# Attention and two feed-forward layers: one copy per product group out of PSUM, its halves joined by a DMA and GpSimd, and other waits in the first pair

## What is computed

```python
# q, k, v: (2, 8, 768, 64) f32; proj: (64, 6)
q_bits = (einsum('bhsd,dk->bhsk', q, proj) > 0); k_bits likewise
mask   = q_bucket[:, :, :, None] == k_bucket[:, :, None, :]   # same 6 bits
scores = where(mask, q @ k.T / 8, -1e9)
attn   = exp(scores - max); attn = attn / (sum(attn) + 1e-9)
x      = (attn @ v)  -> (1536, 512)            # heads side by side
# feed-forward 1: h = x @ w_in; g = P(h) / (Q(|h|) + 1e-6); x = g @ w_out    (512 -> 2048 -> 512)
# feed-forward 2: h = x @ w_in; g = h - tanh(h);            x = g @ w_out
```

## Time and profile before

| | |
|---|---|
| median of 3 runs | 796.71 us (795.78 to 798.22) |
| profiled execution | 797.45 us, its span 795.6 us, granted clock 0.998 of full |
| busy | PE 773.9 us (97%), DVE 554.8 (70%), ACT 476.3 (60%), POOL 127.3 (16%) |
| DMA | 56.54 MB, mean 71 GB/s; nearly all of it issued by SyncE |
| chain that ended last | PE 73%, DVE 16%, DMA 3%, issue 3% |

### The profile page before, as it was taken

One profiled execution on the slowest core, in us unless ns is written; L12 is line 12 of the kernel. 1 busy time (PEld: TensorE's weight loads), 2 busy tenths in 40 slices (PEclk: granted clock), 3 DMA queues, 4 the chain that ended last, 5 costly groups with the idle time before them and its releaser, 6 DMA issues.

```text
span 795.6 us, 11859 instructions
## 1 busy us (share of the span) xinstructions
PE 773.9 (97%) x3840; PEld 647.5 (81%) x3840; DVE 554.8 (70%) x895; ACT 476.3 (60%) x921; POOL 127.3 (16%) x112
## 2 busy tenths in 40 slices
PE   5989999999999999999999999999999999999998
PEld 3879899899988777787888888888888888888886
DVE  4869999999997999999888988966442322223222
ACT  3869889889888687877666766755432222222221
POOL 5334524533539200000000000000000000000000
PEclk9999999999999999999999999999999999999999
DMA  5766767677474430000000132320000100001001
GB/s 114 156 159 151 169 152 180 154 168 181 114 182 113 129 124 0 1 2 1 0 1 15 26 102 84 106 81 13 0 1 1 53 1 1 0 1 54 0 1 54
DMA packets 64603, 56.54 MB, mean 71 GB/s; under 512 B 31664, under 2 KB 50352, under 8 KB 64560
## 3 DMA queue, kind: packets, MB, share of 16 engines
q1 hardware_dynamic: 62848, 55.52, 27.5%
q10 hardware_dynamic: 1712, 0.46, 0.3%
HBM read 29.57 MB, written 3.19 MB: 41 GB/s over the span
## 4 chain that ended last, share of the span: by engine, by line
PE 73%; DVE 16%; DMA 3%; issue 3%; POOL 1%; SPq 1%; ACT 1%; DVEq 0%; ACTq 0%; POOLq 0%
PE acc L718 28%; PE h_ps L689 27%; PE slot L232 5%; PE turn_ps L353 5%; PE pv_ps L313 3%; PE pv_ps L315 3%; DVE sqr L824 2%; DVE row_min L501 2%; DVE pol L845 2%; DVE pt_lo L548 2%; DVE pol L837 1%; DMA kA<-k_hot 1%; DVE pol L856 1%; DVE pol L831 1%; DVE wout_lo L885 1%
## 5 line engine op out<-in xcount | busy, mean ns | idle before, releaser
L689 PE MATMUL h_ps<-x_hi,win_lo 128*128 128x512 f32 x384 | 151.6, 395 | 0.0
L689 PE MATMUL h_ps<-x_lo,win_hi 128*128 128x512 f32 x384 | 151.4, 394 | 0.0
L689 PE MATMUL h_ps<-x_hi,win_hi 128*128 128x512 f32 x384 | 151.2, 394 | 0.0
L739 ACT ACTIVATE g_hi<-pol 128x512 fp32r<-128x512 f32 x96 | 60.9, 634 | 129.5 <-PE acc L718 105.3
L869 DVE TENSOR_TENSOR g_lo<-pol,g_hi 128x512 fp32r<-128x512 f32 x96 | 65.9, 686 | 101.4 <-ACT g_hi L739 101.2
L548 DVE TENSOR_TENSOR pt_lo<-turn_ps,pt_hi 128x384 fp32r<-128x384 f32 x192 | 98.0, 551 | 12.1 <-ACT pt_hi L452 10.7
L452 ACT ACTIVATE pt_hi<-turn_ps 128x384 fp32r<-128x384 f32 x192 | 84.2, 490 | 22.9 <-PE turn_ps L353 21.8
L501 DVE TENSOR_REDUCE row_min<-slot 128x1 f32<-128x768 f32 x96 | 90.6, 944 | 6.6 <-PE slot L232 6.6
L428 ACT ACTIVATE E<-slot,row_min 128x768 f32<-128x768 f32 x96 | 87.4, 910 | 2.7 <-DVE row_min L501 2.7
L689 PEld LDWEIGHTS h_ps<-x_lo,win_hi 128*128 128x128 f32 x384 | 72.2, 188 | 16.9
L689 PEld LDWEIGHTS h_ps<-x_hi,win_hi 128*128 128x128 f32 x384 | 72.2, 188 | 16.8
(11 more groups left out here) (105 smaller groups left out, 1367.3 us busy)
## 6 DMA issues: line engine op xcount, KB each, us to landing
win_raw<-in_moe_w_in SPq DMA_DIRECT2D x32, 256.0 KB, 3.1
wout_raw<-in_moe_w_out SPq DMA_DIRECT2D x32, 256.0 KB, 2.8
q_nat<-in_q SPq DMA_DIRECT2D x16, 192.0 KB, 3.4
v_nat<-in_v SPq DMA_DIRECT2D x8, 384.0 KB, 4.6
scale<-softmax_scale SPq DMA_DIRECT2D x16, 192.0 KB, 3.1
qA<-q_hi SPq DMA_DIRECT2D x15, 192.0 KB, 2.5
qB<-q_hi SPq DMA_DIRECT2D x15, 192.0 KB, 3.0
qB<-q_lo SPq DMA_DIRECT2D x15, 192.0 KB, 3.2
```

The lines of the kernel that those rows point to most:

```text
L689: mm = eng.matmul(h_ps[t % 4][:, :], w[:, ws], columns(x, kt, c), start=kt + n == 0, stop=kt == KT - 1 and n == 2)
L739: eng.activation(g_hi[:, t % TEMPS, :], pol[:, t % TEMPS, :], ACT.Copy).then_inc(mlp_sems["g_hi"], 1)
```

## The change

Three parts. **Groups:** every group leaves `pv_ps` in one copy of 128x384, group 1 by VectorE and the others by ScalarE, into a new tile `x_raw[e]`. A DMA moves the half that stands on the wrong partitions into `x_pair` (`shift`), and GpSimd adds the other half to it (`pool_add`), for head 0 at n = 11, for head 1 at n = 3 of the next pair at the head of `pool_x`. For head 1 the high part of v now stands in the second 64 columns. **Queue:** `spread_scale` is split into `scale_out` and `scale_in`, and these and the shifts get new places in `sync_att`. **First pair:** ScalarE instead of VectorE makes the copy `opA[0][1]` of k, the loads of `ca` and `cb` have a semaphore of their own (`coefs`), which only their users wait for, and `cb_abs` moves behind the first exponentials.

```diff
         def act_first(eng):
...
+            eng.wait_ge(loads["t_k"], 2)
+            eng.activation(opA[0][1][0:D, :], turned[1][0:D, :], ACT.Copy
+                           ).then_inc(loads["t_hi_k"], 1)
-            eng.wait_ge(loads["consts"], 16 * N_CONST)
+            eng.wait_ge(loads["consts"], 32)
...
-            eng.tensor_copy(opA[0][1][0:D, :], turned[1][0:D, :]).then_inc(loads["t_hi_k"], 1)
-            eng.tensor_copy(opB[0][1][0:D, :], turned[1][0:D, :]).then_inc(loads["t_hi_k"], 1)
+            eng.tensor_copy(opB[0][1][0:D, :], turned[1][0:D, :]).then_inc(loads["t_hi_kb"], 1)
...
-        def act_pv_low(eng, p, c):
+        def group_free(eng, p, c):
             eng.wait_ge(sems["pv"], BIAS + GROUPS * p + c + 1)
-            eng.wait_ge(sems["x_sum"], BIAS + GROUPS * p + c)
-            eng.activation(pv_low[:, :], pv_ps[D:2 * D, 0:HALF], ACT.Copy
-                           ).then_inc(sems["pv_low"], 1)
+            eng.wait_ge(sems["x_add"], BIAS + 2 * p - 1 + c // 2)
+
+        def act_out(eng, p, c):
+            if c != DVE_GROUP:
+                group_free(eng, p, c)
+                eng.activation(group_at(c), pv_ps[:, 0:HALF], ACT.Copy).then_inc(sems["out_act"], 1)
...
-        def dve_x_sum(eng, p, c):
...
-            eng.tensor_tensor(x_pair[e * D:(e + 1) * D, hf * HALF:(hf + 1) * HALF],
-                              pv_ps[0:D, 0:HALF], pv_low[:, :], ALU.add
-                              ).then_inc(sems["x_sum"], 1)
+        def dve_out(eng, p, c):
+            if c == DVE_GROUP:
+                group_free(eng, p, c)
+                eng.tensor_copy(group_at(c), pv_ps[:, 0:HALF]).then_inc(sems["out_dve"], 1)
...
+        def pool_add(eng, p, e):
+            mine = slice(e * D, (e + 1) * D)
+            for c in (2 * e, 2 * e + 1):
+                done, count = group_out(p, c)
+                eng.wait_ge(done, count)
+            eng.wait_ge(loads[f"shift{e}"], 16 * (p + 1))
+            eng.sem_inc(loads["pool_here"], 1)
+            eng.tensor_tensor(x_pair[mine, :], x_pair[mine, :], x_raw[e][mine, :], ALU.add
+                              ).then_inc(sems["x_add"], 1)
...
-        def pool_x(eng, p):
+        def pool_x(eng, p, done, count):
+            eng.wait_ge(done, count)
+            pool_add(eng, p, 1)
...
+                if n == 11 and not last:
+                    pool_add(eng, p, 0)
...
+                def shift(p, e):
+                    for c in (2 * e, 2 * e + 1):
+                        done, count = group_out(p, c)
+                        eng.wait_ge(done, count)
+                        here()
+                    eng.wait_ge(sems["xn"], BIAS + p)
+                    here()
+                    eng.dma_start(x_pair[e * D:(e + 1) * D, :], x_raw[e][D - e * D:2 * D - e * D, :]
+                                  ).then_inc(loads[f"shift{e}"], 16)
...
                     copy_split(p + 1, 0)
-                    spread_scale(p, 0)
+                    if not is_zero(p):
+                        shift(p - 1, 1)
+                    scale_out(p, 0)
                     load_v(p + 1)
                     copy_hot(p + 1, 0)
+                    scale_in(p, 0)
                     copy_split(p + 1, 1)
                     copy_hot(p + 1, 1)
-                    spread_scale(p, 1)
+                    shift(p, 0)
+                    scale_out(p, 1)
+                    scale_in(p, 1)
...
-                eng.dma_start(ca[:, :], coef_a).then_inc(loads["consts"], 16)
-                eng.dma_start(cb[:, :], coef_b).then_inc(loads["consts"], 16)
+                eng.dma_start(ca[:, :], coef_a).then_inc(loads["coefs"], 16)
+                eng.dma_start(cb[:, :], coef_b).then_inc(loads["coefs"], 16)
...
                 for j in range(EARLY_OUT):
                     load_weight(0, "out", j)
-                spread_scale(PAIRS - 1, 0)
+                shift(PAIRS - 2, 1)
+                scale_out(PAIRS - 1, 0)
+                scale_in(PAIRS - 1, 0)
```

More of the change, by code:

```diff
@@ L67, in build @@
         "pe": ["pt", "pv", "scores0", "scores1", "aux"],
-        "act": ["pt_hi", "exp0", "exp1", "aux_act", "pv_low"],
-        "dve": ["rowmin", "sum", "recip", "aux_dve", "pt_lo", "x_sum"],
-        "pool": ["hi", "lo", "vhi0", "vhi1", "vlo0", "vlo1", "xn", "xhi", "xlo"],
+        "act": ["pt_hi", "exp0", "exp1", "aux_act", "out_act"],
+        "dve": ["rowmin", "sum", "recip", "aux_dve", "pt_lo", "out_dve"],
+        "pool": ["hi", "lo", "vhi0", "vhi1", "vlo0", "vlo1", "x_add", "xn", "xhi", "xlo"],
     }
@@ L75, in build @@
     loads = {name: top.enter_context(nc.semaphore("s_" + name))
-             for name in ["ident", "consts", "ready", "coef", "proj", "q", "k", "v", "out", "ops0", "ops1",
-                          "scale_out0", "scale_out1", "scale_in0", "scale_in1", "pool_here", "sync_here"]
+             for name in ["ident", "consts", "coefs", "ready", "coef", "proj", "q", "k", "v", "out", "ops0", "ops1",
+                          "scale_out0", "scale_out1", "scale_in0", "scale_in1", "shift0", "shift1", "pool_here", "sync_here"]
              + ["t_turn", "t_q", "t_k", "t_dots", "t_bits", "t_hot", "t_hot_q", "t_hot_k",
-                "t_hi_q", "t_hi_k", "t_lo"]
+                "t_hi_q", "t_hi_k", "t_hi_kb", "t_lo"]
              + [f"w_in{j}" for j in range(J)] + [f"w_out{j}" for j in range(J)]}
@@ L143, in build @@
         row_inv = sb(att, "row_inv", [P, 2, T], F32)
-        pv_low = sb(att, "pv_low", [D, HALF], F32)
+        x_raw = [sb(att, f"x_raw{e}", [P, S], F32) for e in range(2)]
         x_pair = sb(att, "x_pair", [P, S], F32)
@@ L213, in exp_done, with group_out @@
             return sems[f"exp{m % 2}"], BIAS + p * T + m // 2 + 1
+        DVE_GROUP = 1
+        def group_out(p, c):
+            if c == DVE_GROUP:
+                return sems["out_dve"], BIAS + p + 1
+            return sems["out_act"], BIAS + (GROUPS - 1) * p + (c if c < DVE_GROUP else c - 1) + 1
         def is_zero(p):
@@ L294, in pe_first @@
             eng.wait_ge(loads["t_hi_q"], 2)
-            eng.wait_ge(loads["t_hi_k"], 2)
+            eng.wait_ge(loads["t_hi_k"], 1)
+            eng.wait_ge(loads["t_hi_kb"], 1)
             eng.wait_ge(loads["t_lo"], 2)
@@ L309, in pe_pv @@
                 eng.wait_ge(sems[f"vlo{e}"], BIAS + p + 1)
-                eng.wait_ge(sems["x_sum"], BIAS + GROUPS * p + c)
+                done, count = group_out(p, c - 1) if c else group_out(p - 1, GROUPS - 1)
+                eng.wait_ge(done, count)
             for kt in range(i * T // G, (i + 1) * T // G):
@@ L404, in act_first @@
                                    ).then_inc(loads["t_hot_k"], 1)
-            eng.activation(cb_abs[:, :], cb[:, :], ACT.Abs).then_inc(loads["coef"], 1)
             for m in range(AHEAD - 1):
                 act_exp(eng, 0, m)
+            eng.wait_ge(loads["coefs"], 32)
+            eng.activation(cb_abs[:, :], cb[:, :], ACT.Abs).then_inc(loads["coef"], 1)
         def staged_free(eng, b):
@@ L555, in dve_att @@
                     dve_step(eng, 0)
-                if last and n == TILES - 2:
-                    dve_x_sum(eng, p, GROUPS - 2)
                 if first and n == 2:
@@ L704, in pe_g2 @@
                 eng.wait_ge(sems["pt_lo"], BIAS + 2 * TILES * PAIRS)
-                eng.wait_ge(sems["x_sum"], BIAS + GROUPS * PAIRS)
+                done, count = group_out(PAIRS - 1, GROUPS - 1)
+                eng.wait_ge(done, count)
             for i in range(4):
@@ L1008, in spread_scale, with scale_in @@
                                   ).then_inc(loads[f"scale_out{e}"], 16)
+                def scale_in(p, e):
                     eng.wait_ge(loads[f"scale_out{e}"], 16 * (p + 1))
@@ L1080, in _ @@
                     load_weight(0, kind, j)
-                spread_scale(PAIRS - 1, 1)
+                shift(PAIRS - 1, 0)
+                scale_out(PAIRS - 1, 1)
+                scale_in(PAIRS - 1, 1)
+                shift(PAIRS - 1, 1)
                 eng.wait_ge(sems["pv"], BIAS + GROUPS * PAIRS)
@@ L1136, in _ @@
                 dve_att(eng, PAIRS - 2, turn=False)
-                eng.wait_ge(loads["coef"], 1)
+                eng.wait_ge(loads["coef"], 2)
+                eng.wait_ge(loads["coefs"], 32)
                 eng.wait_ge(loads["ready"], 2)
```

37 lines of the change are left out of this document (18 added, 19 removed).

## The result

The changed kernel takes **814.68 us** (median of 4 runs, 813.45 to 815.09) against 796.71: a ratio of 1.0215 (95% interval 1.020 to 1.023). Slower was forecast, but by 10, to 807; it is 18, and 1.7 above the range. The profiled execution took 814.42 with a span of 812.6, which is 17.0 longer than the span of before. I go through it in the order of the prediction.

The account below looks back on a forecast made before the run. TensorE paces attention, VectorE the first feed-forward chunk, then TensorE, so the feed-forward start passes on one for one. h_ps 8.6 later, plus 1.0 holds and 0.4 clock, is 10.0 on 797.45: 807.4, said 807; range 799.5 to 813.

Parts of the forecast that it names:

- the ring: Attention loop: second copy_split waits via scale_in for x_norm, addition and shift, queued behind the first copy_split; 31.2 us a pair.
- from above three such holds (4.5); I take 1: Behind the first h_ps: GpSimd's added additions lengthen VectorE's operations; 1 taken, upper value 4.5.
- the lower clock 0.4: Behind the first h_ps: TensorE's lower clock after its wait for the first weight adds 0.4.
- the last shift 4.2 to landing: Tail: after six weight loads, the last shift lands in 4.2, at 33.0 after pair 6's first copy_split issue.
- S to C: From first issue of copy_split(p+1,0) (S) to that of copy_split(p+1,1) (C), through shift, addition, x_norm: 14.1.
- A lower clock costs nothing there either.: Attention loop: TensorE's lower clock adds nothing to a pair, since the ring has no TensorE work in it.
- plus 1.6 at the lower clock: + 38.8: Last pair: lower clock adds 1.6, TensorE alone reaching h_ps 38.8 after pair 6's first copy_split issue.
- seventh in a burst, 4.1 to landing: Attention loop: the shift, issued seventh in its burst, lands in 4.1; bounds 2.5 to 4.7.
- The rival that it lands as if alone: Rival: the shift lands like a burst's first copy, so the time is 799 to 801; chance 0.08.
- 1.8 + 3.5 + 1.6 in pair 0: Pair 0 gains: earlier first scores 1.8, rest of 5.3 from no kA<-k_hot wait 3.5, no lower clock 1.6.
- Rival C: Ring as forecast, but more VectorE-GpSimd holds and a late weight load at the hand-over: over 813; chance 0.08.
- The rival that the ring is hidden, 784: Rival: TensorE keeps the pace, 13 less at feed-forward start, 0.5 back; needs a ring under 27.7; chance 0.09.

Follow-up runs that it names:

- e5: Changed kernel with the last shift of pair 6 issued ahead of the six early weight loads instead of behind them: 809.6 us.
- e15: Kernel before with only the scale's two transfers at their new queue places; no shift, sums and first pair as before: 791.3 us, ratio 0.9912.
- e8: Changed kernel without GpSimd's two additions for the last pair: 812.8 us, ratio 1.0183 to the kernel before.
- e16: Changed kernel with 20 useless matmuls added on TensorE ahead of its wait for the first weight: 814.3 us, ratio 1.02 to the kernel before.
- e9: Changed kernel with scale_in behind the second copy_split and copy_hot, and GpSimd's head-0 addition behind k_lo: 798.9 us, ratio 1.0016 to the kernel before.

## Why the prediction was right in its direction and wrong in its size

The mechanism was right and the ring's size too. The step that failed is the hand-over: "from above three such holds (4.5); I take 1" and "the lower clock 0.4" put 1.4 behind the first `h_ps`, and the runs show 5.3; ahead of it "the last shift 4.2 to landing" was 6.0, which brings the first weight 1.8 later. Of the 7.0 by which the span's 17.0 exceeds the sum's 10.0, the ring has 1.2, the tail 1.8 and the stretch behind `h_ps` 3.9.

- **"This closes a ring."** Right, in place and size: 31.3 a pair for 31.2, S to C 13.5 to 14.3 (14.1), C to the preparation 9.7 to 10.3 (9.5), the preparation 7.4 to 7.5 (7.5), the addition 1.8 to 1.9 (1.8), TensorE waiting 1.0 to 3.6 for `kA<-k_hot` (2 to 3.5). Opened at either of two places it lets go, and shortened at a third it shortens. S of pair 6 was 1.2 later than the forecast 214.2: 0.7 from the first S, 58.91 for 58.2, and 0.5 from five rings.
- **"A lower clock costs nothing there either."** Right within the ring: two of the five waits have a slow stretch behind them, and the two rings concerned, 30.9 and 32.0, show no common cost (the others have 31.0 to 31.5). But the 1.6 for the lower clock in the last pair ("plus 1.6 at the lower clock: + 38.8") was not there: TensorE stayed at the full clock behind 3.63 and was ready for `h_ps` 37.6 after S, so that it waited 6.3 and not 3.
- **The shift "seventh in a burst, 4.1 to landing"** was 3.6 to 4.4. The rival that it lands as if alone, 2.5, fell; with it falls, for a transfer in a burst, the estimate of 2.45 from the Trainium skill ("DMA: Bandwidth & Descriptors", the anatomy of one DMA). Where nothing stood just ahead of it, the trace agrees with that estimate: the last shift of the changed kernel landed in 2.5, that of e5 in 2.7.
- **The start, "1.8 + 3.5 + 1.6 in pair 0".** The first scores came at 13.51 (13.8), but the wait for `kA<-k_hot` in pair 0, which was to go, was 3.17 at 43.92: `k_hot` was issued 3.0 earlier, not 4, and landed 3.9 earlier, but TensorE was ready for it 4.5 earlier as well (40.75 for 45.21), which the step left out. The row:

```profile
43.92 0.58 PE L242 MATMUL slot<-kA,qA 128*128 128x384 f32 x2 [3.17 <-DMA kA<-k_hot]
```

- Of the start and the queue's new order, only the latter was worth having (e15).
- **"The last shift 4.2 to landing."** Too small: 6.0, and 0.3 to the addition. I had taken the landing of a seventh copy in a burst, and this one stood behind 1.5 MB of weights. With it the first weight was ready 43.8 after S instead of 42.0, and `h_ps` came 11.7 late where the sum had 8.6.
- **"From above three such holds (4.5); I take 1", "the lower clock 0.4".** The step that failed most: 5.3 instead of 1.4. The two additions that I counted have 1.9 (e8); left out was that the later GpSimd comes to its last work, the more of VectorE's work stands beside it, its `x_norm` and split too. Both upper values together, 4.9, would have been nearly right. Taking the slow stretch behind the wait away gave 0.5 of the stretch (e16). Rival C, "ring as forecast, but the hand-over worse", at 0.08, is what happened.
- **The rival that the ring is hidden, 784.** e9 makes its condition true, and the time is 798.9. Its price was wrong in three terms: the start's 1.8 isn't there, the group waits are 0.4 to 0.7 a pair for 0.93 (in all, TensorE is ready for `h_ps` 9.4 earlier, not 13), and where 0.5 was to be lost behind that, the wait for the first weight takes 4.7 and the stretch 5.2. Without the ring the change would still have gained nothing.
- **The bounds.** S of pair 6 fell within those of the ring. The bounds added up to 815 (and to 797 below, not 798), and the range stopped at 813. For the hand-over the 4.5 of the holds was written down and not added even there, and the landing behind the weights had no bound of its own. That is where the 1.7 above the range comes from.

## What to carry to other kernels

Before moving a wait on an in-order queue, walk round it: what is behind the waiting issue, who waits for that, and does the chain come back to the wait. A ring's length is the sum of its parts whatever the engines' busy shares say, and a step put into it is paid once an iteration (here 1.4 us for an addition of 1.85). Work that is free in a loop because its engine idles there isn't free in the last iteration: where GpSimd and VectorE meet at a hand-over, cost it at each operation that it stands beside. And a gain ahead of a fixed wait is only a longer wait: the best part of this change was the place of one transfer in the queue (e15).
